# A chunked delta-rule attention under two feed-forward layers: joining blocks of inverses ahead of use, and outputs written by dimension through memory

## The reference

```python
def _attn_ref(q, k, v, beta):              # 4 x 8 heads, 768 tokens, 48 dimensions
    k_n = k / (np.linalg.norm(k, axis=-1, keepdims=True) + 1e-06)
    for t in range(S):
        y[:, :, t] = einsum('bhd,bhde->bhe', q[:, :, t], state)
        v_old = einsum('bhde,bhd->bhe', state, k_n[:, :, t])
        state = state + bt * einsum('bhd,bhe->bhde', k_n[:, :, t], v[:, :, t] - v_old)
...
x = attn_out.transpose(0, 2, 1, 3).reshape(3072, 384)
h = maximum(x @ w_in, 0);  x1 = (h * h) @ w_out              # w_in 384 x 2048
out = (silu(x1 @ w_gate) * (x1 @ w_val)) @ w_out2            # w_gate 384 x 1536
```

## Time and profile before

| | |
|---|---|
| median of 3 runs | 1049.47 us (1049.29 to 1050.03) |
| the profiled execution's own time | 1047.97 us |
| its span, first to last instruction | 1046.3 us |
| PE busy | 990.5 us, 95% of the span |
| DVE, ACT, POOL busy | 408.2, 303.0, 208.1 us |
| granted TensorE clock | 1.0 of 2.4 GHz throughout |

### The profile page before, as it was taken

How to read it: one execution, slowest core, us unless ns; L and a number is a source line. 1 busy time by engine, 2 the same in 40 slices (tenths; PEclk the granted TensorE clock), 3 DMA queues, 4 the chain that set the end, 5 groups by cost and what they waited for, 6 DMA issues and landing times.

```text
span 1046.3 us, 24211 instructions
## 1 busy us (share of the span) xinstructions
PE 990.5 (95%) x10752; PEld 823.0 (79%) x10752; DVE 408.2 (39%) x693; ACT 303.0 (29%) x599; POOL 208.1 (20%) x337
## 2 busy tenths in 40 slices
PE   2189999999999999999999999999999999999998
PEld 2178899788778878878888888888888888888887
DVE  3965644434434434543256521322312311322222
ACT  2225333333323333332245411221212211212121
POOL 1186381028307703820000000000000000000000
PEclk9999999999999999999999999999999999999999
DMA  7656423431452052130044010100100100100000
GB/s 232 189 151 197 143 74 86 131 95 53 110 154 63 26 152 80 52 107 23 2 173 145 15 61 1 50 11 1 61 1 1 61 1 1 61 1 0 31 1 31
DMA packets 74392, 73.88 MB, mean 71 GB/s; under 512 B 53168, under 2 KB 53296, under 8 KB 74288
## 3 DMA queue, kind: packets, MB, share of 16 engines
q1 hardware_dynamic: 68624, 64.99, 21.0%
q10 hardware_dynamic: 5664, 7.34, 2.2%
HBM read 56.59 MB, written 15.73 MB: 69 GB/s over the span
## 4 chain that ended last, share of the span: by engine, by line
PE 83%; POOL 8%; DVE 3%; DMA 3%; issue 1%; SPq 1%; ACT 0%; ACTq 0%; POOLq 0%; DVEq 0%
PE bank L895 82%; POOL tinv L399 4%; POOL prod L396 4%; DVE first_tinv L399 1%; DVE first_prod L396 1%; SPq L415 1%; DMA k_sq<-in_ky 1%; DMA inv_scratch<-tinv 1%; POOL tri L390 0%; DMA k_dim<-in_kt 0%; DMA tri_scratch<-gram 0%; DMA first_tri<-tri_scratch 0%; DVE h_lo L856 0%; PE bank L1024 0%; DMA inv<-inv_scratch 0%
## 5 line engine op out<-in xcount | busy, mean ns | idle before, releaser
L895 PE MATMUL bank<-x_hi,w_hi 128*128 128x512 f32 (+1 forms) x768 | 295.3, 384 | 1.2 <-DVE x_lo L831 1.2
L895 PE MATMUL bank<-x_lo,w_hi 128*128 128x512 f32 (+1 forms) x768 | 289.6, 377 | 0.0
L895 PE MATMUL bank<-x_hi,w_lo 128*128 128x512 f32 (+1 forms) x768 | 289.4, 377 | 0.0
L895 PE MATMUL bank<-h_hi,w_hi 128*128 128x512 f32 (+1 forms) x552 | 210.7, 382 | 2.6 <-DVE h_lo L856 2.5
L895 PE MATMUL bank<-h_hi,w_lo 128*128 128x512 f32 (+1 forms) x552 | 204.8, 371 | 0.0
L895 PE MATMUL bank<-h_lo,w_hi 128*128 128x512 f32 (+1 forms) x552 | 204.8, 371 | 0.0
L874 DVE TENSOR_TENSOR stage<-bank,stage 128x512 f32<-128x512 f32 x72 | 49.8, 692 | 318.5 <-ACT stage L741 318.5
L895 PEld LDWEIGHTS bank<-x_hi,w_hi 128*128 128x128 f32 x768 | 145.2, 189 | 29.4 <-DVE x_lo L831 1.6
L895 PEld LDWEIGHTS bank<-x_hi,w_lo 128*128 128x128 f32 x768 | 145.2, 189 | 26.5
L895 PEld LDWEIGHTS bank<-x_lo,w_hi 128*128 128x128 f32 x768 | 145.4, 189 | 24.9
L850 DVE TENSOR_TENSOR stage<-stage,bank 128x512 f32<-128x512 f32 (+1 forms) x112 | 68.4, 611 | 224.3 <-ACT stage L715 224.2
(11 more groups left out here) (84 smaller groups left out, 576.6 us busy)
## 6 DMA issues: line engine op xcount, KB each, us to landing
w_raw<-in_w SPq DMA_DIRECT2D x12, 576.0 KB, 3.8
k_dim<-in_kt SPq DMA_DIRECT2D x12, 512.0 KB, 4.7
q_dim<-in_qt SPq DMA_DIRECT2D x12, 512.0 KB, 3.8
k_prep<-in_kt SPq DMA_DIRECT2D x10, 512.0 KB, 4.2
x1s<-in_w ACTq DMA_DIRECT2D x12, 384.0 KB, 4.7
k_sq<-in_ky SPq DMA_DIRECT2D x12, 384.0 KB, 3.7
v_tok<-in_vy SPq DMA_DIRECT2D x12, 384.0 KB, 4.0
x_scratch<-x1s SPq DMA_DIRECT2D x18, 256.0 KB, 3.1
```

The source lines that it names most:

```text
L895: return pe.matmul(dst, lhsT, rhs, start=start, stop=stop, **kw)
```

## The change

Three things are done together.

1. For tiles 1 to 5 the block of the inverse below the diagonal is computed ahead. POOL, after its solve, copies the inverses with rows and columns exchanged into `tri`. SP stores that (flip_scratch) and loads both kinds of inverse into free quarters of the gram tiles (load_cross, 12 DMAs for a tile). N1 and N2, two PE stages for each tile, multiply 32 x 32 blocks: gram by inverse, then inverse by that. ACT and DVE empty them, and N2 lands in the upper quarter of `inv`. U then gives the whole u, and Z and DZ are gone for chunks 2 to 11.
2. The grams are taken two tiles ahead (G of tile t + 2 in unit t), and the solves' due slots and SP's list change with that.
3. From chunk 2 on, Y is computed with dimensions on partitions, stored to memory by SP (store_y, 2 DMAs), and loaded as rows of features (load_x). The transposes X are gone for tiles 1 to 5; x_hi and x_lo are made from SBUF by three rows of 512 instead of four of 384.

The plan:

```diff
             if u == 0:
 ...
                put(24, "sq", 4)
                put(24, "KS", 2)
-                put(26, "QK", 2)
-                put(27, "lane", 2)
-                put(28, "U", 2)
-                put(30, "Z", 2)
+                put(26, "N1", 1)
+                put(28, "N2", 1)
+                put(30, "QK", 2)
                 put(31, "root", 4)
-                put(32, "DZ", 2)
+                put(32, "U", 2)
             elif u == 1:
                 put(1, "Y", 2)
                 put(3, "DS", 2)
                 put(3, "scale", 3)
+                put(4, "lane", 2)
                 put(5, "KS", 3)
                 put(6, "QK", 3)
                 put(8, "U", 3)
-                put(11, "Z", 3)
-                put(14, "DZ", 3)
-                put(16, "Y", 3)
-                put(18, "DS", 3)
+                put(10, "G", 6)
+                put(12, "Y", 3)
+                put(15, "DS", 3)
+                put(18, "G", 7)
 ...
                 if t < NIT:
+                    if t == 2:
+                        put(2, "N1", t)
                     if p < NIT:
-                        put(0, "G", p0)
-                        put(10, "G", p1)
-                        put(16, "lane", p)
+                        put(6 if t == 2 else 1, "lane", p)
+                        put(32, "N1", p)
+                    if t + 2 < NIT:
+                        put(9, "G", 2 * t + 4)
+                        put(14, "G", 2 * t + 5)
+                    put(4, "N2", t)
-                    chain(n0, dict(KS=2, QK=4, U=5, Z=7, DZ=9, Y=11, DS=12))
-                    chain(n1, dict(KS=14, QK=15, U=17, Z=19, DZ=21, Y=23, DS=24))
+                    chain(n0, dict(KS=2, QK=5, U=7, Y=10, DS=12))
+                    chain(n1, dict(KS=15, QK=16, U=18, Y=21, DS=23))
-                    for g in range(4):
-                        put(30 + g // 3, "X", t, g)
+                    for kc in range(KC):
+                        put(31 + 2 * (kc > 0), "X", t, kc)
```

POOL, the new loads, and SP's list around tiles 1 and 2 and at the tail of the units from 2 on follow. store_inverses now also waits for POOL's flip and stores it with 2 DMAs. load_inverses issues the 12 DMAs of load_cross and then the 8 of before. load_ktok(n2) waits for DS of chunk n1, and load_x(n) for store_y(n):

```diff
+                pool.tensor_copy(tri[:, :, :], tinv[:, :, :].rearrange("p c i -> p i c")).then_inc(flipped, 1)
 ...
+        def load_cross(eng, t, s):
+            block = gram[(2 * t + s) % GRAMS]
+            for bp in range(2):
+                at = lanes(s, 1) + bp * 16
+                eng.dma_start(block[bp * C + HALF:bp * C + C, :, :, HALF:C].rearrange("c r m i -> c (r m) i"),
+                              inv_dram[t, at:at + 16, :].rearrange("m (c i) -> c m i", i=HALF)
+                              ).then_inc(blocks_loaded[s], 16)
+            for x in range(2):
+                for r in range(2):
+                    at = lanes(s, 0) + (x ^ r) * 16 + 8 * r
+                    eng.dma_start(block[x * C:x * C + HALF, r, :, HALF:C],
+                                  flip_dram[t, at:at + 8, :].rearrange("m (i c) -> i m c", c=HALF)
+                                  ).then_inc(blocks_loaded[s], 16)
 ...
             store_both(4)
             store_inverses(1)
             load_q(2)
-            load_inverses(1, 0)
-            load_inverses(1, 1)
+            load_inverses(1)
+            store_both(5)
+            load_triangles(2)
             load_prep(6)
             load_ktok(2)
             load_ky(4)
-            store_both(5)
-            load_triangles(2)
 ...
             for u in range(2, NIT):
 ...
                     load_q(n2)
                     load_ktok(n2)
+                store_y(n1)
+                if p < NIT:
+                    load_ky(2 * p + 1)
+                load_x(n1)
+                if p < NIT:
                     store_inverses(p)
-                    load_inverses(p, 0)
-                    load_inverses(p, 1)
+                    load_inverses(p)
+                if g < NIT:
+                    load_triangles(g)
```

More of the change, by code:

```diff
@@ L143, in program @@
         inv_stored = sem("inv_stored")
+        flipped = sem("flipped")
+        flip_stored = sem("flip_stored")
+        blocks_loaded = [sem(f"blocks_loaded{s}") for s in range(2)]
+        cross_filled = sem("cross_filled")
+        cross_ready = [sem(f"cross_ready{x}") for x in range(2)]
+        whole_filled = sem("whole_filled")
+        whole_ready = [sem(f"whole_ready{ab}") for ab in range(2)]
         first_stored = [sem(f"first_stored{i}") for i in range(3)]
@@ new lines, in store_inverses, with load_inverses @@
+                for s in range(2):
+                    at = slice(lanes(s, 0), lanes(s, 0) + HALF)
+                    sp.dma_start(flip_dram[t, at, :], tri[at, :, :].rearrange("p s t -> p (s t)")
+                                 ).then_inc(flip_stored, 16)
+            def load_inverses(t):
+                sp.wait_ge(inv_stored, 16 * t)
+                sp.wait_ge(flip_stored, 32 * t)
+                for s in range(2):
+                    load_cross(sp, t, s)
+                for s in range(2):
+                    if t == 1:
+                        sp.wait_ge(dz_filled, s + 1)
+                    else:
+                        sp.wait_ge(u1_filled, 2 * t + s - 1)
+                    for i in range(2):
+                        load_blocks(sp, t, s, i)
@@ new lines, in store_x1, with store_y @@
+            def store_x1(u):
+                c, c0, w = UNITS[u]
+                for kc in range(KC):
+                    sp.wait_ge(x1_copied[kc], u + 1)
+                    sp.dma_start(x1_dram[kc, :, c * T + c0:c * T + c0 + w], x1s[:, kc, c0:c0 + w]).then_inc(x1_stored, 16)
+            def store_y(n):
+                for ready in y_ready:
+                    sp.wait_ge(ready, 2 * (n + 1))
+                for ab in range(2):
+                    sp.dma_start(y_dram[n].rearrange("(h d) (b x t) -> x d b h t", d=D, b=2, t=C)[ab],
+                                 y_dim[ab * C:ab * C + D, :, :, :, :].rearrange("d b a r t -> d b (a r) t")
+                                 ).then_inc(y_stored, 16)
@@ L548, in _ @@
             load_ky(5)
+            store_x1(0)
             load_q(3)
             load_ktok(3)
+            store_y(2)
             load_v(4)
             load_k(4)
+            load_x(2)
+            load_prep(7)
+            store_both(6)
             load_q(4)
             load_ktok(4)
+            store_y(3)
+            load_prep(8)
+            store_both(7)
+            load_x(3)
             store_inverses(2)
-            load_inverses(2, 0)
-            load_inverses(2, 1)
+            load_inverses(2)
+            load_triangles(3)
             for u in range(2, NIT):
-                t, p = u, u + 1
+                t, p, g = u, u + 1, u + 2
                 n1, n2 = 2 * t + 1, 2 * t + 2
[L563 to L566, removed]
+                store_x1(u - 1)
                 load_v(n1)
@@ L665, in run @@
                     store_triangles(act, n, 1)
+                elif name == "N1":
+                    act.wait_ge(cross_filled, n)
+                    for bp in range(2):
+                        act.activation(cross_rows(n, 0, bp), bank_rows(BANKS[stage_][bp], 0), ACT.Copy, scale=-1.0
+                                       ).then_inc(cross_ready[0], 1)
+                elif name == "N2":
+                    act.wait_ge(whole_filled, n)
+                    take_whole(copy, stage_, 0)
                 elif name == "fetch":
@@ L805, in run @@
                                           mask[:, :].unsqueeze(1).to_broadcast([P, 8, C]), ALU.mult).then_inc(qk_ready, 1)
+                elif name == "N2":
+                    dve.wait_ge(whole_filled, n)
+                    take_whole(copy, stage_, 1)
+                elif name == "N1":
+                    dve.wait_ge(cross_filled, n)
+                    for bp in range(2):
+                        dve.tensor_scalar(cross_rows(n, 1, bp), bank_rows(BANKS[stage_][bp], 1), -1.0, None, ALU.mult
+                                          ).then_inc(cross_ready[1], 1)
                 elif name == "KS":
@@ L984, in q_state @@
                                     m = 8 * bp + 2 * a + ab
+                                    if n > 1:
+                                        at = (4 * bp + a) * C
+                                        mm(pair[r ^ flip][dims(ab), at:at + C], state[dims(r), m, :], q_dim[dims(r), m, :],
+                                           start=(flip == 0 and a == 0), stop=False, skip_group_check=True)
+                                        continue
                                     at = (4 * bp + a) * D
```

180 lines of the change are left out of this document (142 added, 38 removed).

## The result

The changed kernel takes 1074.79 us (median of 4 runs, 1074.12 to 1075.93) against 1049.75 us of the kernel before in the same comparison (4 runs): a ratio of 1.0232, 95% interval 1.0217 to 1.0246. It is slower, as forecast, but by 25.0 us where 5.4 were worked out, and 8.8 us above the top of the range.

A forecast was written before the change was run, and what follows sets the result against it. PE was taken as the bound, busy 990.5 of 1046.3 us. PE's saving -23.0, waits +13.7 and +11.4, slot 32 +3.3 gave +5.4 on 1049.47: 1054.9 us, range 1044 to 1066.

The forecast's parts named there:

- Units 2 to 4: N1 at slot 32: N1 waits for late blocks (0.3 us) and its emptying delays h_lo (0.8): 3 x 1.1 = +3.3 us, bounds 1 and 15.
- SP is late in every unit: Rival: store_y lands in 8 us instead of 4, N1 at slot 32 waits 4 us in three units: +12, 1066.9; chance 0.12.
- Y ... saves 0.44 us: Y on PE, weights of 48 columns: 0.44 us per chunk, ten chunks 4.4; taken as -4.0, nearer DS's row, bounds -4.4 and 0.
- Z, DZ and the transposes: Stages dropped from PE: Z and DZ for ten chunks, -25.8 us; transposes for five tiles, -8.2 us.
- N1 and N2: New PE stages of 128 instructions: 1.5 us each, ten stages +15.0 us, bounds 14 and 23.5.
- small blocks cost as much as larger ones: Rival: N1 and N2 take 2.35 us each: +8.5, 1063.4 in all; chance 0.10.
- the floor of 25 ns from start to start: Skill's price whatever the columns: a stage of 128 takes 3.45 us, total 19.5 us more; 0.02 of the small-blocks rival's chance.
- First wait: Late unit 0: the load of k_sq is issued later in SP's list and holds ACT and PE: +13.7 us, bounds 11 and 18.
- Second wait: Start of unit 2: N1 of tile 2 waits for solve, flip and load_cross: +11.4 us, bounds 8 and 17.
- one wait is absent: Rival: a load lands in time; 1041.2 without the first wait, 1043.5 without the second; chance 0.15.

The follow-up runs named there:

- its own experiment: Changed kernel with store_inverses(p) issued between store_y and load_x of the second chunk in SP's list, units from 2 on: 1063.53 us.
- the experiment with idle matmuls: Changed kernel with 90 unused matmuls put into PE's first wait and 25 into the second, to keep the clock from falling: 1073.25 us.

## Why the prediction was wrong

The direction, the two places and the sizes of the two large waits held. Two steps failed and two terms were absent, and all of it pointed the same way.

- **"Units 2 to 4: N1 at slot 32", +3.3 us: mis-sized.** These units lost 12.7 us, of which its own experiment gives back 8.1. The step took 2.8 us for the flips to land, from rows of stores of 128 KB, and had no term for the inverse's own store of 512 KB ahead of them; behind it they took 4.8 to 5.3. That alone turns the wait of 0.3 into one of 2.3 to 2.8 (measured 2.87, 2.81 and 1.70). The step gave 0.8 us to the late h_lo; in units 2 and 3 the group behind N1 lasted some 1.7 us longer, at a granted clock of 0.57, and in unit 4, where the clock stayed up, only 0.3. And it had nothing for the 0.64 us that QK waits for N2's emptying. The rival *SP is late in every unit* had the size (+12) with another cause: it blamed the store of Y, which landed in 4 us as assumed.
- **A term was absent: what a wait leaves behind.** A wait was priced at its length. Behind the first, some 2.7 us went by the lower clock. Around the second, the two halves of N1 took 2.16 us instead of 1.29, and behind it came the slow KS and the group after it: in the kernel with only slot 32 mended, unit 2 is 1.4 us longer than unit 3, with the same stages in both. These sums are read from the starts of matmuls; the experiment with idle matmuls, meant to test them, did not keep the clock up.
- **A second term was absent: N2's emptying ahead of h_lo in unit 0**, 1.34 us. It is no leftover of the first wait, since without that wait it was 2.31.
- **"Y ... saves 0.44 us": wrong.** From the last wide matmul ahead of Y to the first behind it are 2.63 us before (297.15 to 299.78) and 2.56 after (327.92 to 330.48), 0.07 us: the bound at which streaming binds, 0, was near, and the value by DS's row was not. Ten chunks give 0.7, not 4.0.

What held:

- Z, DZ and the transposes: the last stretch is 5.8 us shorter against 6.1 forecast. There is some luck in it: Y gave 0.7 us less there than forecast, and the 0.77 us that the kernel before waits at U of chunk 10 are gone.
- N1 and N2: 128 small matmuls in 1.2 to 1.3 us at full clock, 1.45 with the hand-over, against 1.5. The rival *small blocks cost as much as larger ones* is out. 128 in 1.29 us are 10 ns each. So the floor of 25 ns from start to start that the prediction quoted from the Trainium skill (TensorE: Matmul & The Clock Gate, Back-to-back issue gap and the section before) is contradicted by this row too.
- First wait: 13.6 us more than before against 13.7. That it is so close is luck, because single steps were off both ways: the flip 2.06 instead of 1.5, its stores 3.7 instead of 2.4, the twelve loads of blocks 7.6 instead of 6.8, and from the first store of triangles to their load 4.5 instead of 6.9.
- Second wait: 11.8 against 11.4, with other parts: 10.1 us for the loads, and 1.7 for the bank of N1, which no term had.

PE's saving is then 25.8 + 8.2 + 0.7 - 14.5 = 20.2 us instead of 23.0. With 13.6 + 1.3 + 2.7 for the first place, 11.8 and 0.9 + 1.4 for the second and its slow stretches, 12.7 for units 2 to 4 and 1.2 of a later start, the sum is 25.4; less the 0.77 that are gone at U of chunk 10, 24.6 against 26.1 measured. Some 1.5 us stay open, about 1.0 of them between chunks 3 and 4. Of the 12.7 us 7.4 are waits at N1 and 1.6 waits at QK; the rest lies mostly in the groups behind N1 (10.6, 10.7 and 9.5 us from its second half to the next KS). How that rest splits between late h_lo, bank and clock was not tried apart.

The rival *one wait is absent* shows its worth in reverse: without the first wait the time was 1061.3 (I gave 1041.2), because all that I had left out was still there.

## What to carry to other kernels

When a change shortens the bounding engine and lengthens a chain on others, write the slack of every chain down first: here PE's saving of 20 us was worth nothing until POOL's solve began earlier, N1 got another slot and several items of SP's list changed places, and then the same code won 15 us. Take the landing of a store from its place in the queue and what was issued just ahead of it, not from a row where it went alone. Price a wait of several microseconds with what follows it, and when a load is only consumed late, look at what stands ahead of it in its queue before anything else.

## What the runs showed of the hardware

- The two stores of 128 KB had landed 2.5 us after the first issue when 2 us lay between them and the store of 512 KB ahead (201.62 to 204.10), 3.7 us in unit 0 (99.32 to 103.00), and 4.8 to 5.3 us when the store of 512 KB and a load of 384 KB or a store of outputs went right ahead of them (373.59 to 378.87, and the same place in the other units).
- 128 matmuls with 32 rows and 32 columns of weights and 32 columns streamed took 1.29 us, 10 ns each.
- With weights of 48 columns instead of 64 and 64 columns streamed instead of 48, Y's 128 matmuls took 0.07 us less in all; the saving by fewer columns of weights that DS shows is not there when more columns are streamed.
- After idle stretches of PE the granted clock was 0.50: matmuls of 256 columns then started 0.21 us apart instead of 0.12, 64 small matmuls of 32 x 32 took 1.08 us instead of 0.75, and KS 1.96 instead of 1.15. Idle matmuls ran at 1.0 up to 126, and after 4.18 us without work behind them PE took up again at 0.50. Behind waits of 2.87 and 2.81 us the clock was 0.57 in the next 4 us, behind one of 1.70 us it was 1.0.
- A subtraction on DVE from two tiles in SBUF took 1.02 us beside a busy POOL and 0.65 beside an idle one, and POOL's product of 207 columns took 1.08 us there and 0.58 in the kernel before.
